# Attention with heads on partition halves, values by key pairs and turns two units late, in front of two feed-forward layers

## The reference

```python
# q, k, v: batch 4, heads 8, seq 576, head_dim 64; factor 4
q_d, k_d, v_d = means over 4 neighbouring positions      # 144 positions
out_up = repeat(softmax(q_d k_d^T / 8) v_d, 4)
mask = abs(i - j) < 4
out_local = softmax(where(mask, q k^T / 8, -1e9)) v
x = (out_up + out_local) as (2304 tokens, 512)
h = x @ w_in                  # 512 x 2048
x = (h * tanh(softplus(h))) @ w_out       # 2048 x 512
h = x @ w2_in                 # 512 x 1024
s = h * softmax(h); ln = (s - mean) / sqrt(var + 1e-6) * g_ln
out = ln @ w2_out             # 1024 x 512
```

## Time and profile before

| | us |
|---|---|
| three runs | 763.81, 774.91, 775.99 |
| median | 774.91 |
| the profiled execution | 762.27 |
| its span, first to last instruction | 760.5 |
| TensorE busy | 713.3 |
| VectorE busy | 335.9 |
| ScalarE busy | 231.1 |
| GpSimd busy | 105.3 |

### The profile page before, as it was taken

How to read it: one execution, slowest core, us unless ns; L and a number is a source line. 1 busy time by engine, 2 the same in 40 slices (tenths; PEclk the granted TensorE clock), 3 DMA queues, 4 the chain that set the end, 5 groups by cost and what they waited for, 6 DMA issues and landing times.

```text
span 760.5 us, 12244 instructions
## 1 busy us (share of the span) xinstructions
PE 713.3 (94%) x5120; PEld 648.2 (85%) x5120; DVE 335.9 (44%) x656; ACT 231.1 (30%) x477; POOL 105.3 (14%) x140
## 2 busy tenths in 40 slices
PE   3877777999999999999999999999999999999997
PEld 2655555899999999999999999999878888888886
DVE  4799999633322321222232122222864444444442
ACT  2454545422221121112112111212643343343332
POOL 5677775000000000000000000000200000000000
PEclk8899999999999999999999999999999999999999
DMA  9798995000000000000000000002300000000001
GB/s 239 201 233 225 228 232 119 1 1 1 1 1 0 1 1 1 1 1 1 0 1 1 1 1 1 1 0 75 147 15 28 15 28 16 28 15 28 28 15 41
DMA packets 33701, 37.48 MB, mean 49 GB/s; under 512 B 23024, under 2 KB 23024, under 8 KB 33648
## 3 DMA queue, kind: packets, MB, share of 16 engines
q1 hardware_dynamic: 33648, 36.71, 17.9%
HBM read 31.99 MB, written 4.72 MB: 48 GB/s over the span
## 4 chain that ended last, share of the span: by engine, by line
PE 84%; DVE 10%; ACT 3%; issue 2%; DMA 1%; POOL 0%; SPq 0%; POOLq 0%; DVEq 0%
PE psum L483 26%; PE psum L497 25%; PE psum L579 12%; PE psum L555 10%; PE psum L404 2%; PE psum L458 2%; DVE pprob L828 2%; PE psum L565 2%; PE psum L420 2%; PE psum L469 2%; DVE mx L815 2%; DVE prob L818 2%; ACT pprobT L636 1%; PE psum L414 1%; DVE wlo L913 1%
## 5 line engine op out<-in xcount | busy, mean ns | idle before, releaser
L882 DVE CAST ghi<-g_sb 128x384 fp32r<-128x384 f32 x96 | 34.5, 359 | 277.9 <-PE psum L497 221.0
L671 ACT ACTIVATE g_sb<-psum 128x384 f32<-128x384 f32 x96 | 47.0, 490 | 307.4 <-PE psum L483 307.4
L483 PE MATMUL psum<-xhi,whi 128*128 128x384 f32 x384 | 129.4, 337 | 1.7 <-DVE xlo L862 1.7
L483 PE MATMUL psum<-xlo,whi 128*128 128x384 f32 x384 | 129.0, 336 | 0.0
L483 PE MATMUL psum<-xhi,wlo 128*128 128x384 f32 x384 | 129.0, 336 | 0.0
L497 PE MATMUL psum<-ghi,wlo 128*128 128x384 f32 x384 | 129.0, 336 | 0.0
L497 PE MATMUL psum<-glo,whi 128*128 128x384 f32 x384 | 129.0, 336 | 0.0
L497 PE MATMUL psum<-ghi,whi 128*128 128x384 f32 x384 | 129.0, 336 | 0.0
L483 PEld LDWEIGHTS psum<-xhi,whi 128*128 128x128 f32 x384 | 72.2, 188 | 2.3 <-issue 2.2
L483 PEld LDWEIGHTS psum<-xlo,whi 128*128 128x128 f32 x384 | 72.2, 188 | 0.0
L497 PEld LDWEIGHTS psum<-ghi,wlo 128*128 128x128 f32 x384 | 72.2, 188 | 0.0
(11 more groups left out here) (99 smaller groups left out, 936.3 us busy)
## 6 DMA issues: line engine op xcount, KB each, us to landing
wraw<-w_dram SPq DMA_DIRECT2D x24, 512.0 KB, 6.7
qT<-qT_dram SPq DMA_DIRECT2D x16, 288.0 KB, 3.1
kT<-kT_dram SPq DMA_DIRECT2D x16, 288.0 KB, 4.2
v<-v_dram SPq DMA_DIRECT2D x16, 288.0 KB
out_dram<-ob SPq DMA_DIRECT2D x18, 256.0 KB, 2.0
vw<-v_dram SPq DMA_DIRECT2D x32, 128.0 KB, 4.8
vw<-v_dram SPq DMA_DIRECT2D x32, 32.0 KB, 4.7
gln<-gln_dram SPq DMA_DIRECT2D x1, 4.0 KB, 2.3
```

The source lines that it names most:

```text
L483: ins = nc.tensor.matmul(bank, a[:, w], b[:, kdx, :], start=(kdx == 0 and n == 0), stop=(kdx == KD - 1 and n == 2))
L671: nc.scalar.activation(g_sb[:, f % HR, :], psum[:, HB1 + f % HB, 0:N1], ACT.Mish).then_inc(g_ok, 1)
L882: nc.vector.tensor_copy(ghi[:, f % GR, :], g_sb[:, f % HR, :]).then_inc(ghi_ok, 1)
```

## The change

- **Local blocks.** Still 10 blocks, now named by (i, jp): `first_query = PSTEP * i + QB * jp`. In the scores the head chooses the partition half and jp the bank, so a row of `prob` holds one head's two neighbouring blocks; turned, the keys of block (i, 0) lie on the lower half and those of (i, 1) on the upper. `vw` holds windows by key pairs: `[P, 2, NP, P]`, both heads side by side, loaded by four DMAs of 512-byte runs where four of 256-byte runs were.
- **Two units late.** With LATE = 2 the turns, copies and value products of unit u run in iteration u+2, on all engines. GpSimd's iteration u ends with pool_values(u-1) where pool_values(u+1) stood. The keys of odd units are pooled on VectorE (`pool_keys`), the rest stays on GpSimd.
- **Normalisation.** One addition and one reciprocal serve both attentions (`denominators`). The pooled probabilities are scaled on ScalarE, in three instructions.
- **Adding up.** VectorE copies the local result to `xy` (`evict_local`, two per unit). The pooled result goes to `od`, and is added when a token tile is about to be split (`add_pooled`, 24 of 128x384).
- **Weights.** SP loads one block of input weights in every second unit, the output weights after the last windows. The input weights are split in sixteen pieces by hidden block, three (AHEAD) before the first hidden block and the others in token tile 0. `hidden` waits for each piece there.

```diff
                 par = u % 2
-                wait(sp, l_valued, 2 * (u - 1))
+                wait(sp, l_valued, u - 1)
                 v_u = v_d[u]
-                for h in range(2):
-                    rows = slice(h * HD, (h + 1) * HD)
-                    first = v_u[0:KW, rows]
-                    for j0, n, step in ((0, 2, NB - 1), (1, NB - 2, 1)):
-                        stride = window(j0 + step) - window(j0)
-                        src = bass.AP(first.tensor, first.offset + window(j0) * P,
-                                      [[P, KW], [stride * P, n], [1, HD]])
-                        dst = vw[rows, par, j0:j0 + (n - 1) * step + 1:step, :]
-                        sp.dma_start(dst, src).then_inc(ld_vw[par], 16)
-
+                for jp, i0, n in ((0, 0, 1), (0, 1, NP - 1), (1, 0, NP - 1), (1, NP - 1, 1)):
+                    src = bass.AP(v_u.tensor, v_u.offset + window(i0, jp) * P,
+                                  [[P, KW], [PSTEP * P, n], [1, P]])
+                    sp.dma_start(vw[jp * KW:(jp + 1) * KW, par, i0:i0 + n, :], src).then_inc(ld_vw[par], 16)
+
+            def load_weights(c):
+                sp.dma_start(wraw[:, c * WB:(c + 1) * WB], w1_d[c]).then_inc(ld_w[c], 16)
+
+
+            order = [c for half_ in range(2) for c in range(half_, 2 * KD, 2)]
             for u in range(UNITS):
                 par = u % 2
                 wait(sp, l_scored, u - 1)
@@ -291,10 +310,15 @@
                 sp.dma_start(kT[:, par, :], kT_d[u]).then_inc(ld_qk[par], 16)
                 wait(sp, pool_v, u - 1)
                 sp.dma_start(v8[:, par, :], v_d[u].rearrange("(p t) c -> p (t c)", t=8)).then_inc(ld_v8[par], 16)
-                sp.dma_start(wraw[:, u * WB:(u + 1) * WB], w1_d[u]).then_inc(ld_w[u], 16)
                 if u > 0:
                     load_windows(u - 1)
+                if u % 2 == 1:
+                    load_weights(order[u // 2])
             load_windows(UNITS - 1)
+            for c in range(2 * KD, WBLK):
+                if c == WBLK - WLATE:
+                    sp.wait_ge(l_valued, UNITS)
+                load_weights(c)
             sp.dma_start(gln[:, :], gln_d).then_inc(ld_g, 16)
...
                 pool.wait_ge(ld_qk[par], 32 * (u // 2 + 1))
                 wait(pool, p_scored, u - 1)
-                wait(pool, pool_qk, u)
+                wait(pool, pool_q, u)
+                wait(pool, pool_k[0], (u + 1) // 2)
                 halves = half_qk[:].rearrange("p a (i r) -> p a i r", r=2)
-                for a, src in enumerate((qT, kT)):
+                both = ((qT, qd), (kT, kd))[:1 if u % 2 else 2]
+                for a, (src, dst) in enumerate(both):
                     four = src[:, par, :].rearrange("p (i r) -> p i r", r=4)
                     ins = nc.gpsimd.tensor_tensor(halves[:, a], four[:, :, 0:2], four[:, :, 2:4], ALU.add)
                 own(ins)
-                for a, dst in enumerate((qd, kd)):
-                    ins = nc.gpsimd.tensor_tensor(dst[:, par, 0:POOLED], halves[:, a, :, 0], halves[:, a, :, 1],
-                                                  ALU.add)
-                ins.then_inc(pool_qk, 1)
+                for a, (src, dst) in enumerate(both):
+                    nc.gpsimd.tensor_tensor(dst[:, par, 0:POOLED], halves[:, a, :, 0], halves[:, a, :, 1],
+                                            ALU.add).then_inc((pool_q, pool_k[0])[a], 1)
 
             def pool_values(u):
                 par = u % 2
@@ -365,19 +390,18 @@
 
             def normalise_local(u):
                 par = u % 2
-                pool.wait_ge(l_rden, u + 1)
-                nc.gpsimd.tensor_tensor(prob[:, par], prob[:, par],
-                                        rden[:, par].unsqueeze(3).broadcast_to([P, NP, 2, KW]),
+                pool.wait_ge(rden_ok, u + 1)
+                rows = prob[:, par].rearrange("p i b k -> p (i b) k")
+                nc.gpsimd.tensor_tensor(rows, rows, rden[:, par, 0:NB].unsqueeze(2).broadcast_to([P, NB, KW]),
                                         ALU.mult).then_inc(l_norm, 1)
 
-            pool_values(0)
-            for u in range(UNITS):
+            for u in range(UNITS + 1):
                 if u > 0:
                     normalise_local(u - 1)
-                if u + 1 < UNITS:
+                if 0 < u + 1 < UNITS:
                     pool_queries_keys(u + 1)
-                    pool_values(u + 1)
-            normalise_local(UNITS - 1)
+                if u > 0:
+                    pool_values(u - 1)
...
@@ -503,24 +531,21 @@
             pe.wait_ge(identb_ok, 1)
             pe.wait_ge(mask_ok, 4)
             pe.wait_ge(zero_ok, 1)
-            for u in range(UNITS):
-                if u == 0:
+            for u in range(UNITS + LATE):
+                if u >= LATE:
+                    turn_pooled(u - LATE)
+                    turn_local(u - LATE)
+                if u < UNITS:
                     score_local(u)
                     score_pooled(u)
-                else:
-                    score_pooled(u)
-                    score_local(u)
-                    turn_local(u - 1)
-                    value_local(u - 1)
-                turn_pooled(u)
-                value_pooled(u)
-
-
-            pe.wait_ge(l_sub, UNITS)
-            hidden(0, 0)
-            turn_local(UNITS - 1)
+                if u == UNITS + LATE - 1:
+
+                    pe.wait_ge(l_sub, UNITS)
+                    hidden(0, 0)
+                if u >= LATE:
+                    value_pooled(u - LATE)
+                    value_local(u - LATE)
             hidden(0, 1)
-            value_local(UNITS - 1)
...
             def exp_pooled(u):
+                par = u % 2
                 act.wait_ge(p_bias, u + 1)
-                wait(act, p_turned, u)
+                wait(act, p_turned, u - 1)
+                wait(act, rden_ok, u - 1)
                 for b in range(NPB):
-                    ins = nc.scalar.activation(pprob[:, b, :], psum[:, SPB, b * POOLED:(b + 1) * POOLED], ACT.Exp,
+                    ins = nc.scalar.activation(pprob[:, par, b, :], psum[:, SPB, b * POOLED:(b + 1) * POOLED], ACT.Exp,
                                                bias=pbias[:, b:b + 1], scale=SCALE / POOLF ** 2,
-                                               accum_out=pden[:, b:b + 1])
+                                               accum_out=den[:, par, NB + b:NB + b + 1])
                 ins.then_inc(p_exp, 1)
+
+            def normalise_pooled(u):
+                par = u % 2
+                act.wait_ge(rden_ok, u + 1)
+                for b in range(NPB):
+                    ins = nc.scalar.activation(pprob[:, par, b, :], pprob[:, par, b, :], ACT.Copy,
+                                               scale=rden[:, par, NB + b:NB + b + 1])
+                ins.then_inc(p_norm, 1)
...
+            for u in range(UNITS + LATE):
+                if u >= LATE:
+                    copy_pooled(u - LATE)
+                    copy_local(u - LATE)
+                if 0 < u <= UNITS:
+                    normalise_pooled(u - 1)
+                if u == UNITS:
+                    for f in range(AHEAD):
+                        weights_in_high(f)
+                    for c in range(KD):
+                        split_x(0, c)
+                if u >= LATE:
+                    evict_pooled(u - LATE)
+                if u < UNITS:
+                    exp_local(u)
+                    exp_pooled(u)
 
...
+            def sum_local(u):
+                par = u % 2
+                dve.wait_ge(l_exp, u + 1)
+                nc.vector.tensor_reduce(den[:, par, 0:NB], prob[:, par].rearrange("p i b k -> p (i b) k"),
+                                        AX.X, ALU.add).then_inc(l_sum, 1)
+
+            def denominators(u):
+                par = u % 2
+                dve.wait_ge(l_sum, u + 1)
                 dve.wait_ge(p_exp, u + 1)
-                nc.vector.tensor_tensor(pden[:], pden[:], eps[:, 0:NPB], ALU.add).then_inc(p_den, 1)
-                dve.wait_ge(p_den, u + 1)
-                nc.vector.reciprocal(prden[:], pden[:]).then_inc(p_rden, 1)
-                dve.wait_ge(p_rden, u + 1)
-                nc.vector.tensor_tensor(pprob[:], pprob[:], prden[:].unsqueeze(2).broadcast_to([P, NPB, POOLED]),
-                                        ALU.mult).then_inc(p_norm, 1)
-
-            def denominators_local(u):
-                par = u % 2
-                dve.wait_ge(l_exp, u + 1)
-                nc.vector.tensor_reduce(den[:, par], prob[:, par], AX.X, ALU.add).then_inc(l_sum, 1)
-                dve.wait_ge(l_sum, u + 1)
-                rows = lambda x: x[:, par].rearrange("p j h -> p (j h)")
-                nc.vector.tensor_tensor(rows(den), rows(den), eps[:], ALU.add).then_inc(l_den, 1)
-                dve.wait_ge(l_den, u + 1)
-                nc.vector.reciprocal(rden[:, par], den[:, par]).then_inc(l_rden, 1)
-
-            def add_up(u, part):
-                par = u % 2
-                if part == 0:
```

(82 more changed lines are left out.)

## The result

| | before | after |
|---|---|---|
| median of the runs, us | 772.72 (4 runs, 763.81 to 775.99) | 816.06 (4 runs, 814.78 to 818.21) |
| span of the profiled execution, us | 760.5 | 814.5 |
| first feed-forward matmul, us | 135.53 | 188.31 |
| from there to the end, us | 625.0 | 626.2 |

The changed kernel takes 1.060 times as long (95% interval 1.051 to 1.070). The ratio leaves out the slowest run of before, 775.99 us, 1.6% above its fastest, which the medians of 772.72 and 774.91 count in. Of the 54.0 us that the span has grown by, 52.8 lie ahead of the first feed-forward matmul.

What follows compares the result with a forecast made beforehand. Before, a 7.59 us chain per attention unit, VectorE busiest; after, a ring of SP's waits, loads and GpSimd's pooling. First feed-forward matmul 49.0 us later: 762.3 + 49.0 + 0.5 = 811.8, plus 2: 814 us, range 786 to 834.

Steps and rivals of the forecast that it cites:

- The ring: Attention: SP waits for pooled values, issues loads, GpSimd pools, SP is released; one turn per unit, 152.2 us; chance 0.60.
- The length of a turn: Attention, SP to GpSimd and back: 10.6 us without a weight block, 13.0 with one, 11.7 on average.
- the upper bound: SP's four window issues in a turn: at most 3.1 us, half a microsecond for a stalled issue; 2.6 was taken.
- The two ends: Attention before and after the turns: 19.5 us to the start, 12.8 from last release to first feed-forward matmul.
- Behind it: After the first feed-forward matmul: 0.5 us longer, from weight splits in token tile 0; other terms nothing.
- the cold TensorE of the prediction's last rival: Tail and first hidden blocks at half clock after idling: 3 to 6 us more, 817; inside the ring's chance.
- a term put at nothing: Attention products behind the first hidden block: as many as now, so no change in time.
- The sum: Whole kernel: 762.3 + 49.0 + 0.5 = 811.8 us, plus 2 for the fast profiled run: 814.
- The faster case: Attention: ring not closed or shorter than engines' own work, mean turn below TensorE's 6.0; 740 us, chance 0.06.
- The short ring: Attention turns at least values, 8.7 and 10.5 us; first feed-forward matmul at 156, total 783 us; chance 0.18.
- slower by over 2%: Whole kernel against before: chance 0.88, with 0.06 for within 2% and 0.06 for faster by over 2%.

Runs made afterwards that it cites:

- e1: Changed kernel with SP issuing v8 one unit later, its wait for pooled values one GpSimd iteration earlier: 765.23 us, 0.995 of before.
- e3: Changed kernel with GpSimd's iteration u ending in pool_values(u) instead of pool_values(u-1), SP untouched: 762.87 us, 0.994 of before.
- e8: On top of e6, weight block issued ahead of SP's wait for pooled values, and unit 14's pooled eviction ahead of ScalarE's first casts: 748.53 us.
- e6: Changed kernel with q and k of unit u+2 issued from ScalarE instead of SP: 746.79 us, 0.972 of before.
- e5: On top of e1, SP also issues the window loads one unit later: 755.08 us, 0.982 of before.
- e7: Changed kernel with the weight block issued ahead of SP's wait for pooled values instead of behind the windows: 804.17 us.
- e2: Changed kernel with v8 and its old wait issued behind windows and weight block, right before the next q: 781.72 us, 1.016 of before.

## Why the prediction was right, point by point

**The ring.** Forecast as a closed chain with one turn per unit, 13 turns; measured so, with the waits of SP and GpSimd at the places named, and undone by moving either end of it (e1, e3).

**The length of a turn.** By its own terms, in the turn from 69.05 to 79.57: v8 and windows 2.95 (forecast 0.44 + 2.6), q's issue 0.58 (0.38), k from issue to GpSimd's start 3.77 (3.8 + 0.1), GpSimd 3.2 (3.2). Sum 10.5 against 10.6. In the turn with a block: 3.59 to q, 0.42, k 4.54, GpSimd 4.2: 12.8 against 13.0. Over all turns the means are 10.89 and 13.45; the 13 together took 156.9 us (17.61 to 174.55) against 152.2. The mis-sized term is SP's issues. Added up over the 13 turns, with the forecast in brackets: from v8's issue to q's 45.7 us (41.9), q's issue 9.1 (4.9), from k's issue to GpSimd's start 54.3 (56.7), GpSimd 47.5 (47.6), GpSimd's end to v8's issue 0.3 (1.3). In three turns the four window issues took 3.6 or 3.7 us and in three others q's issue 1.0 to 1.6:

```profile
95.29 1.40 SPq L309 DMA_DIRECT2D qT<-qT_dram  x1
...
103.65 3.58 SPq L298 DMA_DIRECT2D vw<-v_dram  x4
```

Such a stall, k's at 30.72, stood in the earlier trace rows and was costed only in the upper bound. k's landing, which varies most (3.1 to 5.7 us), was forecast 2.4 us too long in the sum.

**The two ends.** The first pooled values end at 19.7 (19.5). From the last turn's end at 176.6 to the first feed-forward matmul pass 11.7 us (12.8), by another way than I had it: not the windows of unit 14, but the turn of unit 15 behind ScalarE's casts and its eviction, and VectorE's additions. The number was right there for a partly wrong reason; e8 shows VectorE's row to be as long as ScalarE's. 19.7 + 156.9 + 11.7 = 188.3, measured 188.31, forecast 184.5. That the end came out within 1.1 us is partly luck.

**Behind it.** Forecast 0.5 longer, measured 1.2 (626.2 against 625.0). The weight splits in token tile 0 take 685 ns each, with GpSimd idle as in the earlier trace rows, and hide; the 0.5 forecast for them did not come. The first hidden block ran at half the clock:

```profile
188.00:192.50 4.50, 4.37 (x15) 3.80 (x16) 1.57 (x4) 1.28 (x3) 0.00 (x0) 0.52 0.76 303
192.50:205.00 12.50, 12.50 (x113) 12.24 (x114) 9.54 (x20) 9.07 (x17) 0.00 (x0) 1.00 0.38 128
```

0.52 is 1.2 GHz for nearly all of it, after eight microseconds in which TensorE was busy for 4.27; its twelve matmuls took 4.17 us where four blocks later took 8.52, or 2.1 each. So the cold TensorE of the prediction's last rival went with the ring, and cost about 2 us here, where the rival had 3 to 6. Against before, whose first block took 2.33, it is 1.8 us longer; the value products behind it give 0.6 back (0.81 us where before has 1.37), a term put at nothing. Together that is about the 1.2. In the ring itself the clock cost nothing, since TensorE waited anyway.

**The sum.** 811.8 in the profiled execution's terms (measured 816.28), 814 for the median (816.06). The 2 us added for the spread of before had no counterpart: the changed kernel's runs lie within 3.4 us of each other. They made up for nearly half of the 4.5 us by which the sum fell short, which is luck.

**The rivals.** The faster case (740, chance 0.06) had the right picture of what lies behind the ring: with it open (e6) the period is 6.33 where the rival asked for 6.0, the first feed-forward matmul at 119.39 where I had 113, and 746.79 us come out. The short ring's 783 is only 1.0% above the 774.91 of before, so its 0.18 should not have been counted in the 0.88 for slower by over 2%; the forecast's own sums give 0.70. What was too simple in my picture was that opening the ring at one wait would be enough. The expectations of e1, e3 and e5 rested on that, and the times lie 13, 11 and 5 us beyond the bands of 740 to 752 (e5: 742 to 750).

## What to carry to other kernels

When work is moved by a unit or two in one engine's order, list every wait on its semaphore, and first those in queues that issue transfers: a wait that isn't edited changes its meaning when what it waits for moves. Then write down the closed chains (wait, what is queued behind it, who needs that, who signals) and divide each one's length by the units that it spans; where the largest of these numbers is above every engine's own work, it is the period. Loads that everything needs should stand behind no wait for something that is used late, in a queue of their own if need be.

## What of the hardware was not expected

- The local score products and value products swapped their times. At a granted clock of 1.00, 20 products in 40 records: scores 0.81 us before and 1.38 in e6, values 1.37 before and 0.81 in e6. I had costed this at nothing, which was right for a whole unit (2.18 and 2.19 together). Before, the scores went over all four combinations of row and column halves and the values over the two matching ones; now it is the other way round. In TensorE's instructions in order of time, before:

```profile
62.23 1.37 PE L447 MATMUL psum<-probT,vw 64*64 64x58 f32 x40 [1.02 <-ACT probT L625]
...
67.28 0.81 PE L420 MATMUL psum<-kT,qT 64*64 64x64 f32 x40
```

and in e6:

```profile
73.17 0.81 PE L496 MATMUL psum<-probT,vw 64*64 64x58 f32 x40
...
75.45 1.38 PE L446 MATMUL psum<-kT,qT 64*64 64x64 f32 x40
```

  The Trainium skill (TensorEngine Tiling (Array Packing), Key Properties) says that different tiles can load weights and multiply in parallel; the trace agrees in that the four-way order is 1.7 times as fast as the two-way one. A variant in which both go over all four was not tried.
- The same 288 KB load of k takes a median of 3.2, 4.3, 4.9 or 6.3 us to land (e7, changed kernel, e2, e1), with the order of the issues around it. A longer landing need not be a loss: e6 has a median of 6.2 us (20 to 127 us) and is the fastest kernel, e7 has 3.2 and takes 804.17.
- Window loads of 512-byte runs land in a median of 3.4 us over the stage, where those of before take 4.6 (from 60 to 92 us 3.2, against the 4.9 of the earlier trace rows), and occupy SP for nearly as long as before (2.48 us for four against 2.59 in the earlier trace rows). The Trainium skill (DMA: Bandwidth & Descriptors, Specifications) puts the least transfer for line rate at 512 B; the direction agrees, and how much of it is a less crowded queue no run here tells apart.
